# Loading only the new rows of V for a tile and copying the shared rows on chip by DMA

## The reference

```
k_full = concat([mem_k, k[l_start:r_end]]);  v_full = concat([mem_v, v[l_start:r_end]])
scores = scale * q_c @ k_full.T;  a = exp(scores - max);  a = a / (sum(a) + 1e-9)
out[c] = a @ v_full
```

## Time and profile before

| | us |
|---|---|
| median of 3 runs | 502.53 |
| lowest and highest | 501.0 to 506.43 |
| the profiled execution | 501.95 |
| its span, first to last instruction | 500.0 |

### The profile page before, as it was taken

One profiled execution on the slowest core, in us unless ns is written; L12 is line 12 of the kernel. 1 busy time (PEld: TensorE's weight loads), 2 busy tenths in 40 slices (PEclk: granted clock), 3 DMA queues, 4 the chain that ended last, 5 costly groups with the idle time before them and its releaser, 6 DMA issues.

```text
span 500.0 us, 12964 instructions
## 1 busy us (share of the span) xinstructions
PE 448.6 (90%) x4601; PEld 251.5 (50%) x4602; DVE 212.9 (43%) x890; ACT 268.9 (54%) x464; POOL 184.8 (37%) x147
## 2 busy tenths in 40 slices
PE   2689999999997899886889999999999999999992
PEld 2577777777776543454533434433444344434430
DVE  1798988988988471038421121212121212121110
ACT  1477777776776410103225666757575657565640
POOL 2587887887887210002601131313131313210110
PEclk9999999999999999997779999999999999999998
DMA  9999999999999988999999874101010101010000
GB/s 145 186 251 194 228 280 202 273 280 185 277 276 285 346 275 295 425 431 419 422 408 408 308 256 172 45 22 44 24 45 22 44 24 45 23 43 21 22 2 0
DMA packets 98651, 95.66 MB, mean 191 GB/s; under 512 B 86680, under 2 KB 87128, under 8 KB 95928
## 3 DMA queue, kind: packets, MB, share of 16 engines
q1 hardware_dynamic: 94328, 73.38, 53.1%
q10 hardware_dynamic: 1008, 14.68, 7.6%
q0 software_dynamic: 3280, 7.15, 4.2%
HBM read 88.51 MB, written 7.73 MB: 192 GB/s over the span
## 4 chain that ended last, share of the span: by engine, by line
PE 60%; POOL 18%; issue 8%; DMA 7%; DVE 3%; ACT 2%; SPq 1%; POOLq 0%; ACTq 0%; DVEq 0%
PE bank L897 39%; POOL arena L542 9%; POOL arena L537 8%; DMA arena<-in_moe_w_dram 6%; PE bank L875 6%; PE bank L820 2%; PE bank L676 2%; PE bank L608 2%; PE bank L623 1%; PE bank L844 1%; PE bank L864 1%; PE bank L907 1%; PE bank L686 1%; SPq L427 1%; DMA arena<-in_q_dram 1%
## 5 line engine op out<-in xcount | busy, mean ns | idle before, releaser
L897 PE MATMUL bank<-arena 128*64 (+1 forms) x448 | 198.7, 599 | 2.9 <-issue 2.5
L907 PE MATMUL bank<-arena 128*64 128x512 f32 x448 | 198.8, 599 | 0.0
L897 PEld LDWEIGHTS bank<-arena 128*64 128x64 f32 x448 | 60.1, 138 | 122.3 <-issue 121.7
L1166 DVE TENSOR_SCALAR arena<-bank 128x256 f32<-128x256 f32 x112 | 39.7, 418 | 181.3 <-PE bank L875 112.5
L576 POOL DMA_INDIRECT out_dram<-arena,tok_sorted x28 | 28.3, 1010 | 188.9 <-ACT arena L1329 188.9
L537 POOL TENSOR_TENSOR arena<-arena,row_inv 96x1024 f32<-96x1024 f32 x32 | 60.6, 1893 | 28.7 <-DVE row_inv L988 28.7
L542 POOL TENSOR_TENSOR arena<-arena,row_max 96x1024 f32<-96x1024 f32 x32 | 60.6, 1893 | 12.4 <-DVE row_max L995 12.4
L907 PEld LDWEIGHTS bank<-arena 128*64 128x64 f32 x448 | 60.1, 138 | 0.0
L1329 ACT ACTIVATE arena<-bank,gate_sorted 128x512 f32<-128x512 f32 x28 | 19.2, 687 | 75.9 <-PE bank L907 75.9
L995 DVE CUSTOM_DVE_ANT_0 arena<-bank,masks 96x128 f32<-96x128 f32 x256 | 55.1, 277 | 9.4 <-PE bank L608 9.4
L1349 ACT COPY arena<-arena 128x2048 f32 x27 | 51.2, 1898 | 1.3 <-issue 1.0
(11 more groups left out here) (180 smaller groups left out, 540.6 us busy)
## 6 DMA issues: line engine op xcount, KB each, us to landing
arena<-in_moe_w_dram SPq DMA_DIRECT2D x18, 2048.0 KB, 10.1
arena<-in_moe_w_dram ACTq DMA_DIRECT2D x7, 2048.0 KB, 9.4
arena<-in_moe_w_dram SPq DMA_DIRECT2D x24, 512.0 KB, 7.4
arena<-in_v_dram SPq DMA_DIRECT2D x32, 240.0 KB
arena<-in_q_dram SPq DMA_DIRECT2D x32, 192.0 KB, 4.8
arena<-in_k_dram SPq DMA_DIRECT2D x20, 192.0 KB, 4.4
arena<-in_moe_w_dram SPq DMA_DIRECT2D x2, 1024.0 KB, 9.1
arena<-in_k_dram SPq DMA_DIRECT2D x4, 240.0 KB
```

The lines of the kernel that those rows point to most:

```text
L897: mm(bank[4 + par][0:HR, :], h_t[:, par, lo:lo + HR], w2_all[:, bass.ds(at_w2 * SEG + f * DM, DM)], start=(f == 0), stop=(f == KF - 1))
L907: ins = mm(bank[4 + par][HR:TR, :], h_t[:, par, lo + HR:lo + TR], w, start=(f == 0), stop=(f == KF - 1))
L1166: ins = vec.tensor_scalar(h_t[:, j % 2, 2 * r * 128:(2 * r + 2) * 128].rearrange("p (c a t) -> p a c t", c=2, a=2), bank[r][:, j % 2 * 256 ...
```

## The change

V is loaded as K is: only the rows that the left neighbour hasn't, to the highest of the 120 partitions (`v_in[CTX - rows:CTX]`). The rows that both tiles need are then copied by a DMA from the top partitions of the neighbour's place to the bottom partitions of the tile's own place. Each copy is issued by SP after the V load of the next tile, and SP waits first until the neighbour's V has landed. PE waits for the copy out of a tile's place before it weights that tile, since the count of weighted tiles is what lets SP overwrite the place.

```diff
+        v_kept = [sem(f"v_kept{i}") for i in range(KQV)]
...
+        def kept_landings(b, t):
+
+            per_batch = 16 if t % KQV == 0 else 32
+            uses = t // TPB * per_batch + (16 if t % TPB < KQV or t % KQV == 0 else 32)
+            return uses if b is None else b * per_batch + uses
...
             def load_v(b, t, batch):
 
                 r = t % KQV
-                start = min(max(TQ * (t % TPB) - LEFT, 0), S - CTX)
+                first, rows = k_rows(t)
                 until(sp, weighted, b, t - KQV + 1)
-                sp.dma_start(heads(v_in[0:CTX, r, :]), v_bs[batch, start:start + CTX]).then_inc(v_arrived[r], 16)
+                sp.dma_start(heads(v_in[CTX - rows:CTX, r, :]), v_bs[batch, first:first + rows]).then_inc(v_arrived[r], 16)
                 if t % TPB < KQV:
                     sp.dma_start(heads(v_in[CTX:NK, r, :]), mv_bs[batch]).then_inc(v_arrived[r], 16)
+
+            def keep_v(b, t):
+
+                kept = CTX - k_rows(t)[1]
+                if not kept or (b is None and t < 0):
+                    return
+                sp.wait_ge(v_arrived[(t - 1) % KQV], landings(b, t - 1, 16))
+                sp.dma_start(v_in[0:kept, t % KQV, :], v_in[CTX - kept:CTX, (t - 1) % KQV, :]).then_inc(v_kept[t % KQV], 16)
 
             for t in range(TPB):
                 load_kq(None, t)
                 if t >= KQV:
                     load_v(None, t - KQV, 0)
+                    keep_v(None, t - KQV - 1)
 
             with sp.Fori(1, B) as b:
                 for t in range(TPB):
                     load_kq(b, t)
                     load_v(b, t - KQV, b if t >= KQV else b - 1)
+                    keep_v(b, t - KQV - 1)
...
             for i in range(KQV):
                 load_v(None, NT - KQV + i, B - 1)
+                keep_v(None, NT - KQV + i - 1)
                 sp.wait_ge(kq_turned, NT - KQV + i + 1)
                 quarter(late[0], i)
+            keep_v(None, NT - 1)
...
                     pe.wait_ge(v_arrived[(j - 4) % KQV], landings(b, j - 4, 16))
+                    if (j - 3) % TPB and live(b, j - 3):
+
+                        pe.wait_ge(v_kept[(j - 3) % KQV], kept_landings(b, j - 3))
```

## The result

The changed kernel takes 531.13 us (median of 4 runs, 529.75 to 534.86) against 501.76 us before (4 runs): a ratio of 1.0604, 95% interval 1.0555 to 1.0653, so about 30 us slower. Medians here are over all executions, ratios and intervals leave out those more than 1.5% above the fastest of their kernel. The forecast had the sign, the place and the number of the stalls; the size, 13.4 us, was less than half of what came.

What follows compares the result with a forecast made beforehand. PE, DVE and POOL were taken to set the attention's pace together, DMA close behind. 501.95 + 12.6 (seven stalls) + 0.8 (PE's instructions) = 515.4, given as 515.5 us; range 504 to 532, its own 508 to 524.

Steps and rivals of the forecast that it cites:

- V's smaller load, taken as 0: Attention loads: 20% less V saves 8 us of DMA time, worth 0 to 2.6 us to the kernel; taken 0.
- The copies and SP's wait for V, taken as 0: Attention, SP's queue: 28 copies need 3 to 7 us of DMA time; SP's wait for an earlier-issued V costs nothing.
- PE's new wait in front of W(t): Attention, PE: the copy has two steps from issue to use; seven weight loads each make PE stall, 12.6 us in all.
- W(t): The weighting matmuls of attention tile t on PE; W(8) is that of tile 8.
- Without a weight load the two steps suffice, 6.7 < 8.48: Attention steps without a weight load: the copy lands after 6.7 us, inside two steps of 8.48 us, so no stall.
- The size of a stall, 2.4 - 0.6 = 1.8 us: At each weight load in attention: PE stalls 2.4 us, slack absorbs 0.6, leaving 1.8; seven make 12.6 us.
- rival D: Attention: stalls drop PE's clock to 1.2 GHz for 6 us each, 17 us more, 532 us in all; chance 0.09.
- Rival C: Attention: V's present landing lag stays, 4.2 us a stall, 29.4 in all, total 532 us; chance 0.12.
- PE's extra instructions, 0.8 us: PE in attention: register operations for 28 new waits cost 0 to 2.1 us; taken 0.8 us.
- What follows shifts as a whole: After attention: later weights are issued as attention's buffers come free, so later stages keep their length; nothing gained back.
- The Trainium skill's turn-taking of the queues: DMA engines alternate queues packet by packet, so a lone copy would slip past a weight load, stall near 0.2 us, total 504.

Runs made afterwards that it cites:

- experiment 8: The kernel before, loading only V's new rows and copying nothing (old rows stand in their place): 500.17 us, ratio 0.9971 to before.
- experiment 7: The changed kernel with each copy issued one iteration earlier, SP guarding the overwritten place, PE waiting only for its own tile's copy: 501.66 us, ratio 0.9974 to before.
- experiment 1: The kernel before, V whole and no copies, with PE also waiting before weighting tile t for V of tile t+2: 526.13 us, ratio 1.0442 to before.
- experiment 3: The changed kernel with ACT's weight loads issued one step later, after tiles 1, 5, ... 25: 524.31 us, ratio 1.0405 to before.
- experiment 5: The changed kernel with SP waiting for the copy out of a place, PE only for the copy into its tile's own place: 504.98 us, ratio 1.0053.
- experiment 6: The changed kernel with each copy issued one SP iteration earlier, right behind its own tile's V load; PE's wait unchanged: 508.71 us, ratio 1.0114 to before.
- experiment 2: The changed kernel with 8 idle PE matmuls ahead of the copy wait in every fourth tile's step, the one that stalls: 520.9 us, ratio 1.0349 to before.

## Why the prediction was wrong, and where it was right

- *V's smaller load, taken as 0.* Right within the measurement (experiment 8). Its upper bound of 2.6 us counted one wait twice: of the four waits in the earlier trace rows, the PE one of 0.5 us at 77.21 and a weight load's 0.7 us at 77.17 are the same wait for the same mem_v.
- *The copies and SP's wait for V, taken as 0.* Right: experiment 7 makes all of them and takes the time of before, and SP never waits for V ahead of a copy in the changed kernel's trace. An issue cost SP 0.82 us rather than the 0.5 assumed; it didn't matter.
- *PE's new wait in front of W(t), with two steps where V had four.* Right in mechanism, place and number: seven stalls, each behind ACT's weight load, and none where a load stands beside the first tile of a batch (experiments 1, 3, 5, 6). The packets under 512 bytes fell by 5,792 (86,680 to 80,888), not by 6,144; the rest was not looked into.
- *Without a weight load the two steps suffice, 6.7 < 8.48.* Right: no other step waits.
- *The size of a stall, 2.4 - 0.6 = 1.8 us.* Mis-sized, 12.6 us where the runs show 16.3. The landing was right: the copy came 87.16 - 76.00 = 11.2 us after W(8), forecast 10.9. But the stretches with a stall grew by 2.75 us on average, not 2.4 (sum 19.2), and less is absorbed behind it. How much is can't be read in the changed kernel, where the low clock covers it; with the clock held at 1.00 (experiment 2) the second halves are 2.9 us shorter than before in all, 0.4 a stall instead of 0.6. 19.2 - 2.9 = 16.3.
- *The clock, left to rival D with a chance of 0.09 and so at nothing in the sum.* This is the step that failed. The clock fell after each of the seven stalls, and that cost 14.8 us (experiment 2), 2.1 a stall, close to the 2.4 a stall and 17 in all that D had priced; its total of 532 us is the one that came, and for its own reason. With the 16.3 of the stalls it makes the 31.1 us between W(0) and W(31). The argument against D was that the stage is otherwise full. It was not enough: ahead of the low clock stands a stretch of 3 us in which PE is busy 0.00. Most of that stretch was to be foreseen: 2.4 us of stall stand behind the 0.5 us that PE is idle there anyway. The two errors hang together, as experiment 1's shortest stall of 2.23 us, after which the clock stayed at 1.00, suggests. The cited warning of the Trainium skill ("TensorE: Matmul & The Clock Gate", section "HAM oscillation", its name for this rise and fall of the clock) on gaps in which PE waits for data agrees with the windows (0.50 behind the stall at 84 to 87 us).
- *Rival C, a stall of 4.2 us and 532 us in all.* Its total came too, but not by its mechanism: a stall made its stretch 2.75 us longer and not 4.2, and the clock did the rest.
- *PE's extra instructions, 0.8 us.* Not seen by itself. Experiment 7, which has as many waits, takes 501.66 us and experiment 8, which has neither waits nor copies, 500.17; so copies and waits together cost about 1.5 us at most, as far as the scatter lets one tell.
- *What follows shifts as a whole.* Nearly: the slot experts' matmuls (L761 to L785) took 35.3 us, where the kernel before took 37.5, and the shift fell from 33.2 to 31.0 us there (30.5 at the end). PE waits 0.5 us for their weights (0.47 ahead of 240.91) where it waited 2.5 before (1.46 and 1.06): their loads are a little ahead when the attention takes longer.
- *The start.* W(0) came 2.1 us late: the scores of the third and fourth tile take 2.02 us each, as behind a stall, where before they take 1.12, though the profile gives the clock there as 1.00. Nothing was tried on it; experiments 7 and 8 have W(0) at 29.4 and 29.3 too and are not slower than before over the whole, so it is not charged to the change. That is argued, not shown.
- *The Trainium skill's turn-taking of the queues* ("DMA: Bandwidth & Descriptors", Queues, rings and completion order), weighed as a rule that would save the copy: as argued, it didn't, for a copy with V ahead of it (9.60 us from issue to landing). Experiment 6 moves the copy out from behind the next tile's V, and six of seven stalls go; but it also moves it ahead of the weight load, so which of the two helped isn't told apart.

Experiment 1 took 526 us and the changed kernel 531. From W(0) to W(31) the traces differ by 5.9 us, and 5.0 of them lie in the second halves, where the clock is low: in the 8 us behind W(10) the granted clock is 0.79 in experiment 1 (86 to 94 us) and 0.61 in the changed kernel (87 to 95). So the copies add less than 1 us to the stretches with the stalls, and the rest is clock. Why it comes back later there stays open.

## What to carry to other kernels

When a transfer is put behind another in a queue and an engine waits for it, count the steps from the event that lets it be issued to the step that needs it, and compare that with the longest thing that can stand in the way (here a 2 MB load, 9.4 us), not with its own size. If a wait only guards a buffer against being overwritten, put it on the engine that overwrites (SP, which has time) rather than on the busiest one. And a stall of PE has a second price, the slow steps after it: look in the trace for stretches in which it would be busy not at all, and price them from rows at the low clock before calling it unlikely.

## What was not expected of the hardware

The same bytes in packets of a quarter of the size (512 KB loads for 2 MB loads) cost the kernel before 3.1% (interval of the ratio 1.0214 to 1.0412), with the queue's share of the engines' span going from 7.6% to 10.4%. The edit also spreads the loads over all steps, and the two were not told apart. And 8 idle matmuls a stall made the changed kernel 10 us faster, by keeping the granted clock at 1.00.
